# The h rows of four blocks transposed on TensorE and not by DMA, stores issued behind weight splits, and absent blocks skipped, in a three-layer kernel (attention and two expert layers)

## What is computed

```python
def _moe2_ref(x, w_gate, w1, w2):
    logits = x @ w_gate
    expert_idx = np.argmax(logits, axis=1)
    ...                                   # gate_w: softmax of the logits, at the chosen expert
    for e in range(E):                    # E = 8
        mask = expert_idx == e
        h = np.maximum(x[mask] @ w1[e], 0.0)
        out[mask] = gate_w[mask, None] * (h @ w2[e])
```

## Time and profile before

| | before |
|---|---|
| median of 3 runs | 1148.33 us |
| the profiled execution | 1144.99 us, of which the span is 1143.3 us |
| TensorE, matmuls | 1111.6 us busy, 97% of the span |
| TensorE, weight loads (beside the matmuls) | 973.7 us, 85% |
| VectorE | 584.2 us, 51% |
| ScalarE | 289.7 us, 25% |
| GpSimd | 312.4 us, 27% |
| the chain that ended last | TensorE 90%, DMA 3%, VectorE 3%, issue 2%, GpSimd 1% |

### The profile page before, as it was taken

One profiled execution on the slowest core, in us unless ns is written; L12 is line 12 of the kernel. 1 busy time (PEld: TensorE's weight loads), 2 busy tenths in 40 slices (PEclk: granted clock), 3 DMA queues, 4 the chain that ended last, 5 costly groups with the idle time before them and its releaser, 6 DMA issues.

```text
span 1143.3 us, 19075 instructions
## 1 busy us (share of the span) xinstructions
PE 1111.6 (97%) x6726; PEld 973.7 (85%) x6726; DVE 584.2 (51%) x1150; ACT 289.7 (25%) x429; POOL 312.4 (27%) x191
## 2 busy tenths in 40 slices
PE   9999999999999999999999999999999959998996
PEld 6899888999999999999999998888878848887884
DVE  6445434322222232222223258888565669897996
ACT  3444344331111132111113211111432022032220
POOL 7300000240000033000003301110476758087672
PEclk9999999999999999999999999999999979999999
DMA  9333231410000021000003101100843887388896
GB/s 352 80 102 83 73 73 28 165 58 0 0 0 0 0 92 55 0 0 0 0 0 103 44 29 28 28 20 8 236 134 83 207 182 228 88 215 173 201 227 96
DMA packets 113315, 99.79 MB, mean 87 GB/s; under 512 B 72559, under 2 KB 97263, under 8 KB 113138
## 3 DMA queue, kind: packets, MB, share of 16 engines
q1 hardware_dynamic: 90050, 62.33, 22.5%
q10 hardware_dynamic: 18720, 25.22, 7.9%
q0 software_dynamic: 4496, 11.56, 3.3%
HBM read 73.48 MB, written 10.92 MB: 74 GB/s over the span
## 4 chain that ended last, share of the span: by engine, by line
PE 90%; DMA 3%; DVE 3%; issue 2%; POOL 1%; SPq 0%; ACT 0%; POOLq 0%; DVEq 0%
PE psum L1421 15%; PE psum L1423 14%; PE psum L1422 14%; PE psum L1467 12%; PE psum L1468 11%; PE psum L1469 11%; PE psum L1657 3%; PE psum L1659 3%; PE psum L1658 3%; DMA h_planes_T<-h_planes 2%; PE psum L1349 1%; PE psum L1333 1%; DMA rows<-x_rows,meta 1%; PE psum L1619 1%; POOL weights_r L475 1%
## 5 line engine op out<-in xcount | busy, mean ns | idle before, releaser
L475 POOL TENSOR_TENSOR weights_r<-weights,weights_r 128x1024 fp32r<-128x1024 f32 x96 | 233.2, 2449 | 618.1 <-ACT weights_r L665 616.6
L1421 PE MATMUL psum<-xhi,weights_r 128*128 128x384 f32 (+1 forms) x772 | 260.0, 337 | 0.0
L1423 PE MATMUL psum<-xhi,weights_r 128*128 128x384 f32 (+1 forms) x772 | 257.9, 334 | 0.0
L1422 PE MATMUL psum<-xlo,weights_r 128*128 128x384 f32 (+1 forms) x772 | 257.7, 334 | 0.0
L1467 PE MATMUL psum<-weights_r,hhi 128*128 128x512 f32 x576 | 226.9, 394 | 0.0
L1469 PE MATMUL psum<-weights_r,hlo 128*128 128x512 f32 x576 | 224.7, 390 | 0.0
L1468 PE MATMUL psum<-weights_r,hhi 128*128 128x512 f32 x576 | 224.6, 390 | 0.0
L909 DVE SCALAR_TENSOR_TENSOR hlo<-psum,hhi 128x384 fp32r<-128x384 f32 x192 | 106.5, 557 | 219.3 <-ACT hhi L660 219.3
L660 ACT ACTIVATE hhi<-psum 128x384 fp32r<-128x384 f32 x192 | 94.6, 493 | 481.2 <-PE psum L1423 481.2
L665 ACT ACTIVATE weights_r<-weights 128x1024 fp32r<-128x1024 f32 x88 | 92.8, 1060 | 224.0 <-DMA weights<-in_moe_w 205.9
L1421 PEld LDWEIGHTS psum<-xhi,weights_r 128*128 128x128 f32 x772 | 144.9, 188 | 1.7
(11 more groups left out here) (189 smaller groups left out, 1111.3 us busy)
## 6 DMA issues: line engine op xcount, KB each, us to landing
weights<-in_moe_w SPq DMA_DIRECT2D x48, 512.0 KB, 3.9
weights<-in_moe_w ACTq DMA_DIRECT2D x48, 512.0 KB, 5.1
qkT<-in_qk SPq DMA_DIRECT2D x18, 512.0 KB, 4.1
v_rows<-in_v SPq DMA_DIRECT2D x18, 256.0 KB, 3.4
x_rows<-xfin SPq DMA_DIRECT2D x18, 256.0 KB, 5.0
wg_row<-in_gate_rows SPq DMA_DIRECT2D x1, 2048.0 KB, 7.2
h_planes_T<-h_planes SPq DMA_TRANSPOSE x46, 4.9
rows<-x_rows,meta POOLq DMA_INDIRECT x26, 4.6
```

Of the source, the lines that this page charges most:

```text
L475: gp.tensor_tensor(rounded(set_, 1, c), raw(set_, c), rounded(set_, 0, c).bitcast(F32), ALU.subtract).then_inc(sem("w1_lo" if c < NW // 2 ...
L1421: mm(out_, ahi, bhi, start=(i == 0), stop=False)
L1422: mm(out_, ahi, blo, start=False, stop=False)
L1423: last = mm(out_, alo, bhi, start=False, stop=(i == n - 1))
```

## The change

Three edits:

- Blocks 2 to 5 get their h turned by TensorE, as block 1 does; the DMA's turn begins with block 6 (`FIRST_TURNED`). For blocks 1 to 4 TensorE runs first_product(b+1), transpose_rows(b+2), second_product(b), transpose_h(b+1), so that the second product stands one block behind. The step of the hand-over, two half second products, moves from block 1 to block 5. All semaphore counts of turned blocks shift by the same constant.
- On GpSimd `store_place` comes behind the four lo splits of w2, not ahead of them.
- In the guarded steps the transposition and split of the rows of block b+2 move inside the branch that block b+1 is real, so that they fall away for absent blocks; TensorE's other branch no longer waits for the h of the block and no longer counts two semaphores up.

```diff
+    FIRST_TURNED = 6
...
             def turn_h(b, i):
 
                 sp.wait_ge(sem("hrow_ready"), seq(b) * 2 + i + 1)
-                if b > 2:
-                    sp.wait_ge(h_planes_in[i], 16 * (b - 2))
+                if b > FIRST_TURNED:
+                    sp.wait_ge(h_planes_in[i], 16 * (b - FIRST_TURNED))
...
-            for b in range(2, NB):
+            for b in range(FIRST_TURNED, NB):
                 for i in range(2):
                     turn_h(b, i)
...
                 for u in range(2):
-                    store_place(e0 + u - 2)
                     for c in range(NW // 2, NW):
                         split_lo(1 - u, n0 + NW // 2 + u * NW // 2 + c, c)
+                    store_place(e0 + u - 2)
...
-            part_h(2, 0)
-            part_h(2, 1)
-            take_xT(3)
-
-            assert NR % 2
-            with dve.Fori(1, (NR - 1) // 2) as two:
+            for b in range(1, FIRST_TURNED - 1):
+                take_h(b + 1)
+                take_xT(b + 2)
+                take_result(b)
+                take_hT(b + 1)
+            part_h(FIRST_TURNED, 0)
+            part_h(FIRST_TURNED, 1)
+            take_xT(FIRST_TURNED + 1)
+
+            assert NR % 2 and FIRST_TURNED % 2 == 0
+            with dve.Fori(FIRST_TURNED // 2, (NR - 1) // 2) as two:
...
                     join_h(b, 1)
                     part_h(b + 1, 1)
+                    if ahead:
+                        take_xT(b + 2)
...
-                if ahead:
-                    take_xT(b + 2)
                 finish(b)
...
-            first_product(2)
-            transpose_rows(3)
-            second_product(1, range(0, FT // 2))
-            first_product(3)
-            transpose_rows(4)
-            second_product(1, range(FT // 2, FT))
-            for b in range(3, NR - 1):
+            for b in range(1, FIRST_TURNED - 1):
+                first_product(b + 1)
+                transpose_rows(b + 2)
+                second_product(b)
+                transpose_h(b + 1)
+            for b, fs in ((FIRST_TURNED - 1, range(0, FT // 2)), (FIRST_TURNED, range(FT // 2, FT))):
+                first_product(b + 1)
+                transpose_rows(b + 2)
+                second_product(FIRST_TURNED - 1, fs)
+            for b in range(FIRST_TURNED + 1, NR - 1):
                 first_product(b + 1)
                 transpose_rows(b + 2)
                 second_product(b - 1)
...
                 with pe.If(real > b + 1):
                     first_product(b + 1)
+                    if b + 2 < NB:
+                        transpose_rows(b + 2)
                     second_product(b - 1)
                 with pe.Else():
-                    pe.wait_ge(sem("hrow_ready"), seq(b) * 2 + 2)
-                    pe.sem_inc(sem("l1a_psum"), 1)
-                    pe.sem_inc(sem("l1b_psum"), 1)
                     finish(b - 1)
 
             for b in range(NR - 1, NB - 1):
-                if b + 2 < NB:
-                    transpose_rows(b + 2)
                 spare_step(b)
```

More of the change, by code:

```diff
@@ L441, in _ @@
             for i in range(2):
-                sp.wait_ge(h_planes_in[i], 16 * (NB - 2))
+                sp.wait_ge(h_planes_in[i], 16 * (NB - FIRST_TURNED))
         @block.gpsimd
@@ L1201, in join_h @@
             def join_h(b, i):
-                dve.wait_ge(h_planes_in[i], (seq(b) - 2) * 16)
+                dve.wait_ge(h_planes_in[i], (seq(b) - FIRST_TURNED) * 16)
                 words = h_row_T[:, i * 512:(i + 1) * 512].bitcast(U16)
@@ L1208, in relu_h @@
             def relu_h(b):
-                dve.wait_ge(sem("h_joined"), seq(b) * 2 - 4)
+                dve.wait_ge(sem("h_joined"), (seq(b) - FIRST_TURNED) * 2)
                 vec.tensor_scalar(psum[:, HT_B:HT_B + 2, :], h_row_T[:, :].rearrange("p (i n) -> p i n", i=2), 0.0, None,
@@ L1218, in split_half @@
                 src = psum[:, HT_B + i, :].rearrange("x (r t) -> x r t", t=P)
-                dve.wait_ge(sem("h_turned"), seq(b) - 2)
+                dve.wait_ge(sem("h_turned"), seq(b) - FIRST_TURNED)
                 if i:
```

## The result

| | before | after |
|---|---|---|
| median of 17 runs each, side by side | 1148.03 us (1141.56 to 1160.78) | 1142.20 us (1139.46 to 1144.29) |
| ratio | | 0.9946, 95% interval 0.9926 to 0.9966 |
| profiled execution | 1144.99 us, span 1143.3 us | 1142.45 us, span 1140.8 us |
| TensorE, matmuls | 1111.6 us, 97% | 1118.1 us, 98% |
| VectorE | 584.2 us, 51% | 563.9 us, 49% |

Faster by 5.8 us, where 13.1 were forecast, and 0.2 us above the upper end of the range. Lines of the code have moved: L1421 is L1427 now, L1642 is L1648, L1657 is L1663, L1240 is L1241, L475 is L476, L537 is L538.

A forecast was written before the change was run, and what follows sets the result against it. The second expert layer's time was taken as TensorE's matmuls plus three stalls. Terms -10.7 + 0.4 - 5.0 + 1.0 + 1.5 - 1.3 + 1.0 = -13.1 us gave 1135.2 us from 1148.33, range 1129.5 to 1142.

The forecast's parts named there:

- no new stall: Variant of the sum in which the change causes no new waits: -17.0 us, 1131.3 us.
- part (a): Blocks 2 to 5 turned on TensorE: +3.5 us of transposes, -14.2 us of stall 1, net -10.7 us.
- stall 1: About 924, before block 6's first product: TensorE waits on xTlo behind late DMA turns of h; 14.2 us with clock loss.
- weights of place 2: Loaded only from about 907.3, split ready near 923, needed by block 6 at 926.1 and 928.8: no cost taken.
- Stall 2: About 1044, block 13's second product: TensorE waits for GpSimd's fourth w2 split behind six stores; 5.0 us in all.
- (b): Stores moved behind the w2 splits on GpSimd: removes Stall 2, -5.0 us, but bursts then meet turns of blocks.
- Store bursts on turns: The two inner store bursts delay DMA turns of h, 0 to 3 us each; +1.0 and +1.5 us taken.
- The tail: Last blocks, VectorE the bound: dropping x work of absent blocks gives -1.3 us, the third store burst costs +1.0 us.
- free ride: Rival: the new store bursts cost nothing and the gain is whole, 1131 us; chance 0.15.
- Weights slow: Rival: weights of place 2 as slow as before, block 6's first product nine microseconds late, 1146 us; chance 0.05.
- clock: Rival: 32 transposes on TensorE cost its clock, 2.3 us more per set, +9.2 us, 1144 us; chance 0.03.
- turns late: Rival: turns late at every store burst, 1144 us, with two of them 1140 or so; chance 0.18.

The follow-up runs named there:

- e14: The changed kernel unedited, rerun in the fourth group on another chip: 1130.13 us, ratio 0.9861.
- e9: The kernel before, unedited, traced again in the third group on another chip: 1145.45 us, ratio 0.9961.
- e16: Changed kernel with the run of 15 gathers cut into pieces behind later weight splits: 1134.01 us, ratio 0.9903.
- e18: e16 repeated without further edit on a fifth chip: 1131.76 us, ratio 0.9880.
- e7: Changed kernel with VectorE's steps of blocks 1 to 4 as a loop and the stores ahead of the splits again: 1144.25 us, ratio 0.9975.
- e5: The changed kernel unedited, second trace, in the second group on another chip: 1139.74 us, ratio 0.9937.
- e15: e4 repeated in the fourth group, beside e14: 1129.56 us, ratio 0.9846.
- e1: Changed kernel with its stores ahead of the w2 splits again: 1136.13 us, ratio 0.9897.
- e4: Changed kernel with VectorE's steps of blocks 1 to 4 as a loop of two passes: 1129.57 us, ratio 0.9849.
- e2: The kernel before with only the stores moved behind the w2 splits: 1144.72 us, ratio 0.9990.
- e8: The changed kernel unedited, third trace, in the second group: 1140.68 us from a single execution.
- e3: Changed kernel with gathers of blocks 10 to 24 moving 256 bytes a row, an eighth: 1132.30 us, ratio 0.9859.

## Why the prediction was right or wrong

**What bounds the kernel: right** for the execution that was read. Both stalls lay where they were read, and both went. Without the loss the layer got shorter by 274.7 - 258.5 = 16.2 us against the 17.0 of "no new stall"; those are two single traces, and by medians side by side e14 is 14.7 us under before, with a wide interval (5.6 to 26).

**The step that failed** is "What is late next?" in part (a), which took nothing for anything new on the way to block 6, so that the -14.2 us of stall 1 went into the sum whole. It went through what the *change* makes late: the turn of block 6, the weights of place 2, the bursts. The first two were in time, and the bursts cost TensorE next to nothing in after. What the runs showed in its place is 10.9 us in after (6 to 10.5 us by the layers of its four traces with the loss) in which VectorE and TensorE start late at 903 to 919 with no releaser. The rows could not have given it: in the trace of before TensorE was busy 47.00 of 47 us up to 916, and the loss was not in that execution. What failed before that is the trust in one trace, with 3.3 us for the spread around it. The second trace of before (e9) has no stall 1 to remove: its 7.43 us on xTlo are the loss itself, one block earlier, and 12.9 us in all. There the change can't gain the 14.2 us, but only what the loss costs less in the new order. What the loss is stays open.

**Term by term.**

- Stall 1, -14.2: as a removed wait right (12.3 to 0.4 us), as a gain right where the loss is absent; where it is present, 6 to 10.5 us of loss stand against it in after.
- The h transposes, +3.5: eight take 0.8 us between the start of the first and the next product, 875.32 to 876.11 in e14; right.
- Hand-over at block 6, 0.4: no wait there at all; block 6's first product starts at 925.17 in e14, for the 926.1 forecast, and at 939.84 in after, which is 926.1 with 3.15 of a late layer and the loss of 10.9.
- Weights of place 2, nothing: right; the fourth split ends at 925.4 in e14 (forecast 923) and its half of the product starts at 927.9.
- Stall 2, -5.0: no wait on weights_r in any trace of after (e16 and e18, whose splits stand behind moved gathers, have 1.2 and 1.6 us); on the same chip (b) is worth 4.5 us (e7 against e5, with the loop as a second edit, which in e15 against e14 is worth nothing), and e1 against e4 gives 6.6 by medians, likewise with the loop between them, and four of e1's nine executions are only 2 to 4 us over e4's median. On top of before alone no gain is shown (3 us by medians, e2).
- Store bursts on turns, +1.0 + 1.5: mis-sized, no cost of them is seen in after or e14. After's joins wait 3.6 us for their DMAs in all, in four waits of up to 1.3 (before: 5.03 us at one alone), and TensorE waits for none of them. The Trainium skill's rule of queues taking turns by packets (*DMA: Bandwidth & Descriptors*, "Queues, rings and completion order") would by the prediction's reading have made it 10 us, and the trace of after does not show them.
- The tail, -1.3 + 1.0: TensorE's wait for hTlo is 1.9 us in after and 2.5 in e14, against 2.2; the two instructions are gone, but the wait didn't get shorter by them, and the +1.0 of the third burst isn't seen either. Net near nothing instead of -0.3. The tail is not the same in every trace, though: in e8, the same program, VectorE's join at 1107.63 waits 4.04 us for a turn issued among the stores of the third burst and loads of weights, and TensorE waits 3.9 us for hTlo, which is the case that the prediction feared there.

**The rivals.** Without the loss the free ride came true by the waits. That the time fits as well, 1130.1 for 1131.3, is partly luck: before's median in that series was 1144.8, 3.5 us under the 1148.33 from which the prediction counts. Weights slow, clock and turns late did not: the 1142.2 us that look like "turns late" (1140 to 1144) come from another place. The clock stays at 1.00 through the h transposes of blocks 2 and 3 (868 to 897) and falls only behind the starved stretch. The sign was right. That the range missed by only 0.2 us is luck too: its upper end was set by late turns, which did not come, and no rival stood for a loss that isn't in the trace of before.

## What to carry to other kernels

A wait of one execution need not be the wait of the next: another loss can take its place, at nearly the same total time (274.7 and 274.0 us here), and the change may remove only one of the two. Before the whole length of a wait is booked as gain, take a second trace of the kernel before, from another chip if there is one, and check that the wait stands at the same instruction with the same releaser. Read a surprise in the changed kernel against a repetition of the same kernel on the chip of the experiment first; three variants here (e1, e3, e4) looked like cures and had only met a series without the loss.

## What was not expected of the hardware

In three of six series here (counting the first of after), each on its own chip as far as is on record, VectorE stood 7 to 15 us ahead of one instruction, of which some 4 were a usual wait, and TensorE's matmuls started 0.7 to 2.1 us apart (0.7 to 1.4 in after) in place of 0.23, while GpSimd issued 15 gathers and a store at 1.3 us each; in the others the same program shows nothing. All nine traces with it show it in small at 820 too, beside three indirect DMAs, with 1.95 to 2.53 us; no other trace does. Five or six indirect stores at the same pace left no mark in after; in e7 five stand beside 2.40 and 1.82 us. Beside the two inner bursts VectorE waited at most 1.3 us for a DMA turn in after and 1.7 in e14; in the tail of e8 it waited 4.04.
